# Pooled attention, soft mixture and gated layer on one core: row maxima in single-bank units

## What is computed

```python
def _attn_ref(q, k, v):                      # 4 batches x 8 heads, 1152 keys, width 64
    q_pool = q.reshape(B, H, S // 2, 2, D).mean(axis=3)          # 576 pooled queries
    scores = scale * np.matmul(q_pool, k.transpose(0, 1, 3, 2))  # 576 x 1152
    scores = scores - np.max(scores, axis=-1, keepdims=True)
    attn = np.exp(scores)
    attn = attn / (np.sum(attn, axis=-1, keepdims=True) + 1e-09)
    return np.matmul(attn, v)
```

## Time and profile before

| what | value |
|---|---|
| time, three runs | 740.49, 740.65, 741.43 us, median 740.65 |
| the profiled execution | 741.45 us, span from first to last instruction 739.7 us |
| start, up to the first score product | 18.92 us |
| head 0, up to its weighing | 10.24 us |
| heads up to the weighing of head 30 | 404.23 us |
| from there to the end | 306.3 us |

### The profile page before, as it was taken

One profiled execution on the slowest core, in us unless ns is written; L12 is line 12 of the kernel. 1 busy time (PEld: TensorE's weight loads), 2 busy tenths in 40 slices (PEclk: granted clock), 3 DMA queues, 4 the chain that ended last, 5 costly groups with the idle time before them and its releaser, 6 DMA issues.

```text
span 739.7 us, 17095 instructions
## 1 busy us (share of the span) xinstructions
PE 726.1 (98%) x6375; PEld 541.8 (73%) x6375; DVE 524.3 (71%) x828; ACT 455.1 (62%) x1008; POOL 483.7 (65%) x429
## 2 busy tenths in 40 slices
PE   6999999999999999999999999999999999999997
PEld 5777777777777767777777677434778888888886
DVE  7888888888888888888888847533895555455542
ACT  4677776776777767767767763214665454545453
POOL 1588888888888888888888872212774444444442
PEclk9899999999999999999999999999999999999999
DMA  5123435334334353343443347899301010101011
GB/s 147 41 59 84 122 92 156 103 106 155 88 104 159 90 156 104 98 164 88 124 139 88 96 140 263 299 386 375 138 0 43 1 43 0 43 0 43 0 43 43
DMA packets 51623, 81.83 MB, mean 111 GB/s; under 512 B 14556, under 2 KB 20572, under 8 KB 51548
## 3 DMA queue, kind: packets, MB, share of 16 engines
q1 hardware_dynamic: 51180, 80.37, 34.8%
q10 hardware_dynamic: 368, 0.46, 0.2%
HBM read 75.94 MB, written 4.79 MB: 109 GB/s over the span
## 4 chain that ended last, share of the span: by engine, by line
PE 94%; DVE 3%; issue 1%; POOL 1%; ACT 1%; POOLq 0%; DVEq 0%; ACTq 0%
PE ps L675 20%; PE ps L652 9%; PE ps L982 8%; PE ps L981 8%; PE ps L980 8%; PE ps L620 6%; PE ps L654 5%; PE ps L656 5%; PE ps L658 5%; PE ps L686 3%; PE ps L580 3%; PE ps L970 2%; PE ps L864 2%; PE ps L894 2%; PE ps L585 1%
## 5 line engine op out<-in xcount | busy, mean ns | idle before, releaser
L1067 ACT ACTIVATE probs<-ps 128x576 f32<-128x576 f32 x288 | 183.7, 651 | 45.1 <-PE ps L658 31.4
L1357 DVE TENSOR_REDUCE mx<-ps 128x2 f32<-128x1024 f32 (+1 forms) x160 | 189.4, 1218 | 29.9 <-PE ps L620 27.9
L546 POOL TENSOR_TENSOR g_lo<-g_buf,g_hi 128x384 fp32r<-128x384 f32 x96 | 102.1, 1065 | 100.9 <-ACT g_hi L1242 100.9
L675 PE MATMUL ps<-probs,v_sb 128*64 128x288 f32 x1152 | 146.8, 409 | 0.1
L509 POOL TENSOR_TENSOR p_sum<-p_sum,probs 128x576 f32<-128x576 f32 x93 | 129.1, 1415 | 0.0
L1585 DVE SCALAR_TENSOR_TENSOR v_buf<-u_buf 128x384 f32<-128x384 f32 x96 | 60.4, 629 | 86.4 <-ACT u_buf L1235 85.8
L675 PEld LDWEIGHTS ps<-probs,v_sb 128*64 128x64 f32 x1152 | 79.6, 137 | 56.4 <-issue 5.2
L1235 ACT ACTIVATE u_buf<-ps,half 128x384 f32<-128x384 f32 x96 | 55.7, 581 | 93.9 <-PE ps L970 93.9
L980 PE MATMUL ps<-wo_hi,g_hi 128*128 128x512 f32 x282 | 110.4, 391 | 0.6 <-POOL g_lo L546 0.5
L982 PE MATMUL ps<-wo_lo,g_hi 128*128 128x512 f32 x282 | 110.8, 393 | 0.0
L981 PE MATMUL ps<-wo_hi,g_lo 128*128 128x512 f32 x282 | 110.6, 392 | 0.0
(11 more groups left out here) (216 smaller groups left out, 1252.1 us busy)
## 6 DMA issues: line engine op xcount, KB each, us to landing
pre<-in_moe_w SPq DMA_DIRECT2D x41, 512.0 KB, 4.9
v_sb<-in_v SPq DMA_DIRECT2D x32, 288.0 KB, 2.9
k_raw<-in_k SPq DMA_DIRECT2D x31, 288.0 KB, 3.8
q_raw<-in_q SPq DMA_DIRECT2D x32, 256.0 KB, 4.0
from_x<-in_moe_w SPq DMA_DIRECT2D x9, 512.0 KB, 5.1
p_inv<-inv_dram SPq DMA_DIRECT2D x62, 72.0 KB, 2.7
out<-o_stage SPq DMA_DIRECT2D x34, 128.0 KB, 2.3
staged<-in_moe_w SPq DMA_DIRECT2D x8, 512.0 KB, 5.5
```

The lines of the kernel that those rows point to most:

```text
L675: mm = pe.matmul(ps[D * h:D * h + D, 4, 0:HALF], v_sb[n % 2][:, u, :], probs[:, u, HALF * h:HALF * h + HALF], start=(i == 0), stop=(i == N ...
L1067: nc.scalar.activation(dst, ps[:, b0:b0 + 2, 0:HALF], ACT.Exp, scale=SCORE_SCALE).then_inc(exp_done, 1)
L1357: top = nc.vector.tensor_reduce(mx[0:w, NC * t:NC * t + 2], ps[0:w, b:b + 2, :], AX.X, ALU.max)
```

## The change

The two halves of a job become units of their own. A unit u is one product of 64 rows and 512 columns into one bank (6 or 7 in turn), in array half u % 2, and DVE reduces it with one instruction of 512 columns. A head has units 0 to 7 for the four full tiles, ahead of steps 0 to 7; units 8 and 9 for the last 128 keys (two products in array half 0, three in half 1), both ahead of step 8; and one product `row_max_rest` behind step 8. This last one is for the tile of 64 queries: `q_rest` is 128 x 128 with the 64 queries twice on its diagonal and zeros elsewhere, so that one product of all 128 rows gives 128 output lanes, lanes 0 to 63 with the first half of the keys, lanes 64 to 127 with the second. DVE reduces 128 x 512 there where it reduced 64 x 1024. The two halves of the maxima are joined after they have been turned, by a new DVE instruction (`join_rest`) for which `place_neg_max` now waits; DVE stands at it until PE has turned the maxima. Unit u waits for the maximum of unit u-2.

Banks 4-5 go to the scores: three pairs serve in turn within a head, and step s waits for the exponential of step s-3. In heads 1 to 30 the even steps issue array half 1 first, so that a step begins in the half that the unit ahead of it doesn't use. Keys and queries of heads 2 and up are turned into the score banks. ACT rounds the queries into `q_rest` with two further instructions per head, and `low_q` waits for them. POOL clears q_rest at the start. `weigh` no longer waits for `max_free`.

```diff
+        def unit_bank(u):
+            return 6 + u % 2
...
         def step_bank(n, s):
-            if n == HEADS - 1:
-                return (2, 0, 6)[s % 3]
-            return 2 * ((n + s) % 2)
+            if s % 3 == 2:
+                return 6 if n == HEADS - 1 else 4
+            return 2 * ((n + s % 3) % 2)
...
+            def row_max_rest(m):
+                if m == 0:
+                    pe.wait_ge(max_free, QT - 1)
+                else:
+                    pe.wait_ge(max_free, units_of(m) + UNITS - 2)
+                pe.matmul(ps[:, rest_bank(m), :], q_rest[m % 2][:, :], k_hi[m % 2][:, 0:KP],
+                          start=True, stop=True).then_inc(max_full, 1)
+
+            def row_max(m, u):
+
+                if u == 0:
+                    pe.wait_ge(turn_free, 2 * m + 2)
+                if u >= 2:
+                    pe.wait_ge(max_free, units_of(m) + (u - 1))
+                b, g = unit_bank(u), u % 2
+                if u < 2 * QF:
+                    t = u // 2
+                    mm = pe.matmul(ps[:, b, :], q_hi[m % 2][rows_of(g), P * t:P * t + P], k_hi[m % 2][rows_of(g), 0:KP],
+                                   start=True, stop=True)
+                else:
+                    tiles = (0, 1) if g == 0 else (2, 3, QF)
+                    for i, t in enumerate(tiles):
+                        mm = pe.matmul(ps[:, b, P * i:P * i + P], q_hi[m % 2][rows_of(g), P * t:P * t + P],
+                                       k_hi[m % 2][rows_of(g), KP:KP + P], start=True, stop=True)
                 mm.then_inc(max_full, 1)
...
-                elif NT * n + s >= 2:
-                    pe.wait_ge(exp_done, NT * n + s - 1)
+                if s >= 3:
+                    pe.wait_ge(exp_done, NT * n + s - 2)
...
-                if n + 1 < HEADS:
-                    pe.wait_ge(max_free, JOBS * (n + 1) + JOBS)
...
-                    if n + 1 < HEADS and s in JOB_STEPS and (n > 0 or s > 0):
-                        row_max(n + 1, JOB_STEPS.index(s))
-                    scores(n, s)
+                    if n + 1 < HEADS and (n > 0 or s > 0):
+                        row_max(n + 1, s)
+                        if s == NT - 1:
+                            row_max(n + 1, NT)
+                    scores(n, s, (1, 0) if s % 2 == 0 and 0 < n < HEADS - 1 else (0, 1))
...
+                if n + 1 < HEADS:
+                    row_max_rest(n + 1)
                 if n + 2 < HEADS:
...
+                for g in range(2):
+                    high(q_rest[m % 2][rows_of(g), rows_of(g)], tail_of(m, P, QLAST)[rows_of(g), :])
...
             def place_neg_max(m):
-                act.wait_ge(neg_full, m + 1)
+                act.wait_ge(rest_joined, m + 1)
...
+            def top_of_rows(m, u):
+                dve.wait_ge(max_full, units_of(m) + u + 1)
+                b, g = unit_bank(u), u % 2
+                if u < 2 * QF:
+                    t = u // 2
+                    top = nc.vector.tensor_reduce(mx[:, NC * t + g:NC * t + g + 1], ps[:, b, :], AX.X, ALU.max)
...
+            def join_rest(m):
+                r = D + QT
+                dve.wait_ge(neg_full, m + 1)
+                if m > 0:
+                    dve.wait_ge(neg_free, m)
+                nc.vector.tensor_reduce(rest_neg[0:r, :], ps[0:r, neg_bank(m), 0:P].rearrange("r (g c) -> r c g", g=2), AX.X,
+                                        ALU.min).then_inc(rest_joined, 1)
...
+            def tops(m, invert):
+                for u in range(UNITS - 1):
+                    top_of_rows(m, u)
+                    if u == 7 and invert:
                         invert_sums(m - 2)
+                top_of_rest(m)
                 join_tops(m)
+                join_rest(m)
```

More of the change, by code:

```diff
@@ L88, in soft_moe_chain @@
     p_rest = at("p_rest", [P, SQ], SLOT_AT)
+    q_rest = [at(f"q_rest{i}", [P, P], SLOT_AT + 2304 + 4 * P * i, F32R) for i in range(2)]
+    rest_neg = at("rest_neg", [P, QLAST], SLOT_AT + 2304 + 8 * P)
     BY_PARITY = SLOT_AT + 4096
@@ L465, in _ @@
                                     pattern=[[-1, P]], channel_multiplier=1).then_inc(ident_ready, 1)
+            for i in range(2):
+                zero = nc.gpsimd.memset(q_rest[i][:, :].bitcast(F32), 0.0)
+            zero.then_inc(ident_ready, 1)
             def prepare(m):
@@ L593, in turn, with row_max_first @@
                 mm.then_inc(turned, 1)
[L595 to L597 removed]
+            def row_max_first(j):
+                if j in (0, QF):
                     pe.wait_ge(rounded, 5 if j == 0 else ROUNDS)
[L599 to L608 removed]
+                if j > 1:
+                    pe.wait_ge(max_free, j - 1)
+                b = job_bank(j)
@@ L629, in turn_neg_max, with scores @@
                 pe.transpose(ps[:, neg_bank(m), 0:P], neg_max[:, :], ident[:]).then_inc(neg_full, 1)
-            def scores(n, s):
+            def scores(n, s, halves):
                 if s == 0:
                     pe.wait_ge(neg_free, n + 1)
-                    if n > 0:
-                        pe.wait_ge(turn_free, 2 * min(n + 2, HEADS))
-                if n == 0 and s == 0:
-                    pe.wait_ge(turn_free, 3)
-                if n == HEADS - 1 and s >= 2:
-                    pe.wait_ge(exp_done, NT * n + max(s - 2, 0))
-                elif NT * n + s >= 2:
-                    pe.wait_ge(exp_done, NT * n + s - 1)
+                    if n == 0:
+                        pe.wait_ge(turn_free, 3)
+                if s == 1 and 0 < n < HEADS - 1:
+                    pe.wait_ge(turn_free, 2 * n + 4)
+                if s == 2 and 0 < n < HEADS - 1:
+                    pe.wait_ge(x_read, n)
+                if s >= 3:
+                    pe.wait_ge(exp_done, NT * n + s - 2)
                 b0 = step_bank(n, s)
                 for part in range(4):
-                    for g in range(2):
+                    for g in halves:
                         rows = rows_of(g)
@@ L1398, in top_logits, with tops_first @@
                                         negate=True).then_inc(l_neg_ready, 1)
+            def tops_first():
+                for j in range(QT):
+                    top_of_rows_first(j)
+                top_of_rest(0)
+                join_tops(0)
             def tops(m, invert):
-                for j in range(JOBS):
-                    top_of_rows(m, j)
-                    if j == 3 and invert:
+                for u in range(UNITS - 1):
+                    top_of_rows(m, u)
+                    if u == 7 and invert:
                         invert_sums(m - 2)
+                top_of_rest(m)
                 join_tops(m)
+                join_rest(m)
             low_k(0)
             low_q(0)
-            tops(0, False)
+            tops_first()
             low_ends(0)
+            join_rest(0)
             low_ends(1)
```

153 lines of the change are left out of this document (78 added, 75 removed).

## The result

The changed kernel takes **749.2 us** (median of 4 runs, 748.09 to 749.7) beside 741.04 us (740.49 to 741.58) for the kernel before, measured together: a ratio of 1.0108 [1.0091, 1.0126]. That is 8.2 us slower; 747.8 was forecast, within 736 to 760.

What follows compares the result with a forecast made beforehand. PE, busy 98%, was taken as the bound, with 0.84 us of stall per head. 31 heads x 0.24 = 7.4, less 0.3 at the start, took 740.65 to 747.75 us; forecast's own range 743 to 755, wider 736 to 760.

Steps and rivals of the forecast that it cites:

- The forecast per head: Steady heads: the weighing begins at 8.57 instead of 8.33 us after the first maximum's product, +0.24 us per head.
- The exchange of stalls: Scores part: 0.84 us of exponential waits per head goes; DVE waits come ahead of unit 9 (about 0.6) and turned maxima (0.4).
- the sum: The prediction's addition of durations from profile rows along one head, then over 31 heads (7.4 us) and the start (-0.3).
- The trip through DVE: Unit loop from PE to DVE and back: 0.43 + 0.68 maximum + 0.05 + 0.11 = 1.27 us, as long as two steps.
- What was set at nothing: Behind the weighing: join_rest, low parts, add_pair, ACT's two roundings, SP's and POOL's work, all taken at zero.
- The term for the start: Before the first join: last reduction shorter by 0.53 us, 0.2 of it to join_rest, so -0.3.
- A: Rival at both DVE waits: stalls weigh less and the third bank pair wins, 732 to 738, say 735 us; 16%.
- B: Rival per head: the two effects cancel, +0.05 to -0.05, 740.5 us; 14%.
- C: Rival in the step loop: halves don't slide past each other freely, seven steps add 0.39 per head, 760 us; 11%.
- D: Rival in the step loop: halves don't overlap while a unit runs, 0.9 to 1.1 per head, 770 us; 6%.
- rule and row: Unit 9's three products: rows show loads within a half hidden; by the skill's rule about 0.2 more, 6 us overall.

Runs made afterwards that it cites:

- e5: Changed kernel with the scores' third bank pair taken back, units and their order kept: 776.86 us, 1.0466 of before.
- e1: Changed kernel with all units one step earlier, the first between weighing and adding up of the head before: 745.97 us, 1.0068 of before.
- e2: Changed kernel with the diagonal product and its maximum first of all units, between weighing and adding up: 745.68 us, 1.0063 of before.
- e6: Changed kernel with array half 0 always first in a step's scores: 749.21 us, 1.0093 of before.
- e7: Changed kernel with the diagonal product replaced by two 64-row products and one 64 x 1024 maximum in heads 1 and up: 772.53 us, 1.0411 of before.
- e9: Changed kernel reordered: diagonal product before adding up, units 8 and 9 ahead of step 0, large units ahead of steps 1 to 8: 738.14 us, 0.9952 of before.
- e3: Changed kernel with maxima of units 0 to 7 and the diagonal product reading half the keys (incomplete computation): 730.85 us, 0.9862 of before.
- e4: Changed kernel with diagonal product and unit 8 before adding up, unit 9 alone ahead of step 8: 738.86 us, 0.997 of before.
- e8: Changed kernel with units 0 and 1 side by side before adding up, diagonal product ahead of step 0, others reordered: 739.12 us, 0.9955 of before.
- e10: e9 with maxima of units 0 to 7 and the diagonal product reading half the keys (incomplete computation): 729.09 us, 0.9833 of before.

## Why the prediction held, step by step

The forecast per head was +0.24, and 0.243 came. Where PE has to load weights with nothing beside it, a product's row begins with its load, so I compare loads with loads. The two that waited, on PE's weight loads of the head of after:

```profile
220.14 0.18 PEld L652 LDWEIGHTS ps<-k_hi,q_hi 64*128 64x128 f32 x1 [0.29 <-DVE mx L1405]
...
222.72 0.14 PEld L661 LDWEIGHTS ps<-ident,neg_max 128*128 128x128 f32 x1 [0.37 <-DVE neg_max L1419]
```

Counted from the first unit at 214.39, predicted and measured:

```
                                          predicted   measured
pace of the units, per step                 0.64        0.65     (214.39 to 218.95 in 7 steps)
unit 9, load                                5.75        5.75     (220.14)
scores end                                  6.67        6.74     (221.00 + 0.13)
diagonal product, load                      6.76        6.83     (221.22)
its maximum on DVE starts                   7.30        7.36     (221.75)
join done                                   8.21        8.28     (222.48 + 0.19)
turned maxima, load                         8.26        8.33     (222.72)
weighing                                    8.57        8.59     (222.98)
maximum of 128 x 512                        0.68        0.687, 0.692
```

The steps in turn:

**The exchange of stalls** was right as put: the waits for exponentials are gone, worth 0.84 by the sum and 0.91 by e5, and two waits for DVE stand in their place. Unit 9's load came to the hundredth. What its wait costs is read in two ways that don't quite agree: step 8 from 219.67, with 0.29 for five small products and 0.52 for its scores, would end at 220.48 and ends at 221.13, 0.65 later; e1 gives 0.46 (0.58 less 0.12). The sum had 0.62. At the join it had 0.44; the view of waits has 12.0 us in 30 heads, 0.40, and what reaches the weighing is about 0.36 (under e2). From the end of the scores on every mark is 0.07 late, and the weighing 0.02, as it follows the load of the turned maxima by 0.26 where the sum had 0.31.

**The trip through DVE** was bounded from two sides by rows that didn't show it, and the value taken for the maximum (0.68, by the length of the work, against 0.62 from the nearest row) was the right one: 0.687 and 0.692. With 0.62 the forecast would have been 744.

**What was set at nothing** behind the weighing stayed at nothing: add_up starts 4.52 after it in both kernels. The first score product comes even 0.33 sooner after the weighing (5.15 for 5.48), but that is the pair of 512 columns that no longer stands ahead of it; the first unit itself starts as the pair did.

**Head 0 was mis-sized.** The term for the start was -0.3, and head 0 had the 0.24 of every other. The first weighing came 1.78 late, but in the profiled execution TensorE's granted clock up to the first score product was 0.76, where before had 0.94. In e6, which differs from after only in the order of halves, it was 1.00. The clock stood at the lower of its two levels from 10.7 to 24.3 us in after, from 16.9 to 23.7 in before and from 20.4 to 23.8 in e6. Head 0 of before, then start and head 0 of e6:

```profile
18.95:29.16 10.21, 10.21 (x97) 9.21 (x97) 7.78 (x10) 6.24 (x10) 4.91 (x4) 0.77 0.01 2
```

```profile
0.00:18.59 18.59, 12.05 (x66) 9.09 (x67) 13.51 (x38) 8.27 (x24) 3.91 (x13) 1.00 0.50 151
18.59:29.48 10.89, 10.19 (x95) 8.89 (x95) 8.05 (x15) 6.45 (x11) 5.60 (x5) 0.84 0.01 3
```

The first score product stands at 18.59 for 18.95: -0.36, so the -0.3 held. Head 0 takes 10.89 for 10.21: +0.68 at a clock no worse than before's. PE's weight loads of head 0 in e6 show two waits that the sum had at nothing:

```profile
19.61 0.19 PEld L647 LDWEIGHTS ps<-k_hi,q_hi 64*128 64x128 f32 x2 [0.45 <-DVE k_lo L1368]
...
20.89 0.28 PEld L647 LDWEIGHTS ps<-k_hi,q_hi 64*128 64x128 f32 x1 [0.49 <-DVE mx L1405]
```

In head 0 units 0 and 1 stand together behind step 0 and unit 2 one step later, the same closeness as at units 8 and 9. In after, whose products ran slower there, only 0.17 of the second wait was left, and head 0 took 10.40; its lateness of 1.59 lies ahead of the first score product, where the clock was low.

**The stretch behind head 30** was 0.9 shorter than before's, and this isn't the change either. TensorE of before fell to its lower level once in it, and so did that of e6 (0.50 from 481.2 to 484.6), but not that of after:

```profile
474.20:477.60 3.40, 3.40 (x18) 0.92 (x14) 0.32 (x2) 0.00 (x0) 0.00 (x0) 0.50 1.06 396
```

Of the twelve profiled executions the five with such a fall (before, e2, e6, e7, e9) take 306.3 to 306.8 there, the seven without 305.1 to 305.7. The program of this stretch hardly differs. So 8.2 us came about as +7.3 in the steady heads and +0.9 in two ends whose parts, +1.78 and -0.9, both carry the clock. By e6 against before the ends are worth +0.4 (335.84 for 335.42), with a better clock at the start. From after to e6, 10.2 us more at the lower level made the first weighing 1.46 later; before had 3.4 us more of it than e6, so at its clock about 0.5 comes on top. That estimate, +0.9 for the two ends where the sum had -0.06, is the 1 us by which the total lies above the forecast.

**Rivals.** A (both waits shrink, 735) fell by e1 to e3: the waits stood near the sizes summed. B fell with it. C and D (halves that hinder one another) fell by the pace of 0.65. The small products of unit 9 decide between rule and row where the prediction set them side by side. "TensorE: Matmul & The Clock Gate" in the Trainium skill, part on packing small matmuls, lets a load overlap running products only in another row group, and by it the scores would have ended 0.2 later than summed. Unit 9's products lie in one half and start 0.11 apart (220.31, 220.42), no more than a bare load takes; the scores ended 0.07 later, and the weighing came 0.02 later. The score products say it more sharply: 288 columns are about 0.13 by the 0.23 of 512, and the next product of the same half starts 0.13 later, so its load was hidden behind that half's own product. The trace doesn't bear the rule out here. The other citation, "VectorE: DVE Perf Modes", section on the TRN2 errata, gives by its figures an estimate of 0.66 for a maximum over one bank; the rows have 0.687, and the row decides.

What I missed lay in the experiments' expectations: an early product between weighing and adding up costs 0.43, and two in a row 0.79, more than I gave them, so that e1, e2 and e4 each gained less than expected (745.97 for 740, 745.68 for 738 to 740, 738.86 for 721 to 725). e5, e8, e9 and e10 missed their expectations as well, each time through a wait for a maximum that I had taken to be gone or had not seen; e3, e6 and e7 came out near them.

## What to carry to other kernels

When a buffer becomes smaller and its users more, look for the two places where neighbours stand closer than one round trip (here product, 0.43, maximum, 0.69, and load, 0.16: 1.28 us), and at the last one before the join: here these two cost about 0.5 to 0.65 and 0.4 per head, as much as a third pair of score banks gave (0.91). Before undoing such a change, move its instructions: the same ten units and diagonal product in another order beat both kernels (738.14 us).

## What the runs showed of the hardware

A single product between two differently tiled stretches of PE costs 0.43 us though its 512 columns take 0.23 (e1, e2), and two units in a row, 512 columns and then twice 128, cost 0.79 (e4).

Products of the two row halves are independent down to their order: unit 9's wait held everything behind it until 220.14, but from there a score product written later starts first, since its half is free (220.16 ahead of 220.31), and e6's 749.21 us (749.20 for after) show no worth in the order between halves.

`add_pair`, a sum of two 128 x 576 blocks in SBUF on DVE, changed its length with the order around it and with nothing in itself: 1125 ns after, 1712 in e1, 978 in e4, 789 in e5, 1879 in e7 (means of the groups of DVE). What decides is POOL's addition that is running when it starts. POOL and DVE of after, then of e5:

```profile
221.74 2.78 POOL L527 TENSOR_TENSOR p_sum<-p_sum,probs 128x576 f32<-128x576 f32 x2
...
223.89 1.24 DVE L1447 TENSOR_TENSOR probs<-probs 128x576 f32<-128x576 f32 x1
```

```profile
202.68 4.15 POOL L527 TENSOR_TENSOR p_sum<-p_sum,probs 128x576 f32<-128x576 f32 x3
...
206.84 0.74 DVE L1447 TENSOR_TENSOR probs<-probs 128x576 f32<-128x576 f32 x1
```

In after POOL's ends at 224.52 and `add_pair` at 225.13, 0.61 behind it. In 29 heads each of before, after, e1, e2, e3, e6, e7 and e10 it ends 0.61 to 0.63 behind the POOL addition it started beside (median 0.61 or 0.62 in e4, e8 and e9 too, with exceptions), whether 0.3 or 1.3 of that was left. In e5 it mostly starts just as one has ended, and takes 0.74. So DVE's sum of two SBUF blocks stands until POOL's instruction is through. It is hidden behind the weighing in all of them: in e7, where it is longest, the next head's first score product starts at 5.15, as in after.

The granted clock up to the first score product differed between executions of nearly like kernels (0.76 after, 0.94 before, 1.00 in e6), and between after and e6 the first weighing differed by 1.5 us with it. A fall of 3.4 us to the lower level behind head 30 goes with about 1 us. Where a change is worth 8 us, such terms belong in the range.
